# Expert products as filling, norm steps behind the masks, and separate id and gate regions in a delta-rule attention and expert kernel

## The reference, cut to what matters

```python
k_n = k / (norm(k) + 1e-06)
for t in range(S):
    y[:, :, t] = q_t @ state
    state = state + beta_t * outer(k_t, v_t - state @ k_t)
x = (sigmoid(x @ w_gate) * (x @ w_val)) @ w_out        # 3072 x 384, inner 1536
xn = x / (norm(x) + 1e-06);  en = emb / (norm(emb) + 1e-06)
logits = xn @ en.T / tau;    e = argmax(logits)
gate = softmax(logits)[e] (sum + 1e-09)
out = gate * (relu(x @ w1[e]) @ w2[e])                  # inner 1024
```

## Time and profile before

| what | us |
|---|---|
| median of three runs | 1417.88 (1417.28 to 1418.27) |
| the profiled execution, its own time | 1420.6 |
| its span, first to last instruction | 1418.9 |
| start of stages 0, 1, 2, 3 (first product of L976) | 36.27, 68.57, 97.89, 128.30 |
| stages 4 to 23, from one to the next | 39.09 and 39.20 in turn |
| first transposes of the first expert tile (L1215) | 1041.96 |
| first result of DVE from that tile (L749) | 1064.6 |
| one expert tile | 11.6 |

### The profile page before, as it was taken

One profiled execution on the slowest core, in us unless ns is written; L12 is line 12 of the kernel. 1 busy time (PEld: TensorE's weight loads), 2 busy tenths in 40 slices (PEclk: granted clock), 3 DMA queues, 4 the chain that ended last, 5 costly groups with the idle time before them and its releaser, 6 DMA issues.

```text
span 1418.9 us, 28235 instructions
## 1 busy us (share of the span) xinstructions
PE 1324.7 (93%) x11527; PEld 1098.6 (77%) x11527; DVE 581.6 (41%) x1427; ACT 454.6 (32%) x1004; POOL 437.6 (31%) x472
## 2 busy tenths in 40 slices
PE   4899999999999999999999999999559999999996
PEld 4577999999999999999999999999525555555553
DVE  1555444555555555545555555533401111111111
ACT  1445334443434444444434344342101111111110
POOL 4565322333333333323333233312212222222210
PEclk9999999999999999999999999999779999999999
DMA  4232000000000000000000000005231333311100
GB/s 136 72 98 62 18 18 29 13 29 18 30 18 24 13 29 18 19 29 13 29 18 30 15 24 11 24 2 189 87 125 34 119 118 119 121 39 34 33 27 1
DMA packets 42796, 66.89 MB, mean 47 GB/s; under 512 B 6345, under 2 KB 34929, under 8 KB 42672
## 3 DMA queue, kind: packets, MB, share of 16 engines
q1 hardware_dynamic: 36944, 54.19, 11.8%
q0 software_dynamic: 5728, 10.91, 2.6%
HBM read 55.29 MB, written 11.16 MB: 47 GB/s over the span
## 4 chain that ended last, share of the span: by engine, by line
PE 87%; DVE 6%; issue 2%; POOL 2%; ACT 1%; DMA 1%; SPq 0%; POOLq 0%; DVEq 0%
PE ps L1065 23%; PE ps L1228 12%; PE ps L1238 11%; PE ps L1077 8%; PE ps L976 6%; PE ps L1000 3%; PE ps L1030 3%; PE ps L1038 3%; PE ps L1003 2%; DVE MP L550 2%; PE ps L1247 2%; PE ps L1036 2%; PE ps L992 2%; PE ps L960 1%; PE ps L1012 1%
## 5 line engine op out<-in xcount | busy, mean ns | idle before, releaser
L1065 PE MATMUL ps<-xh,wgh 128*128 128x256 f32 x864 | 267.8, 310 | 0.0
L1065 PE MATMUL ps<-xl,wgh 128*128 128x256 f32 x864 | 243.5, 282 | 0.0
L1065 PE MATMUL ps<-xh,wgl 128*128 128x256 f32 x864 | 243.0, 281 | 0.0
L374 POOL TENSOR_TENSOR gl<-sg,gh 128x256 fp32r<-128x256 f32 x144 | 105.8, 735 | 408.2 <-ACT gh L815 408.1
L1228 PE MATMUL ps<-W,xsT 128*128 x372 | 170.2, 608 | 1.9 <-issue 1.0
L1238 PE MATMUL ps<-W,hT 128*128 x496 | 165.1, 486 | 0.9 <-ACT hT L928 0.9
L1065 PEld LDWEIGHTS ps<-xh,wgh 128*128 128x128 f32 x864 | 164.1, 190 | 1.7
L1065 PEld LDWEIGHTS ps<-xl,wgh 128*128 128x128 f32 x864 | 164.7, 191 | 0.5
L1065 PEld LDWEIGHTS ps<-xh,wgl 128*128 128x128 f32 x864 | 163.9, 190 | 0.0
L1238 PEld LDWEIGHTS ps<-W,hT 128*128 128x128 f32 x496 | 94.2, 190 | 73.0 <-issue 15.5
L573 DVE TENSOR_TENSOR sg<-sg,ps 128x256 f32<-128x256 f32 x144 | 60.5, 420 | 216.7 <-ACT sg L811 216.7
(11 more groups left out here) (183 smaller groups left out, 2435.8 us busy)
## 6 DMA issues: line engine op xcount, KB each, us to landing
W<-w_dram SPq DMA_DIRECT2D x16, 1536.0 KB, 11.3
kin<-kv_dram SPq DMA_DIRECT2D x24, 192.0 KB, 2.4
kqT<-qT_dram SPq DMA_DIRECT2D x48, 96.0 KB, 2.5
vin<-kv_dram SPq DMA_DIRECT2D x24, 192.0 KB, 2.3
x_dram<-x2r SPq DMA_DIRECT2D x24, 192.0 KB, 2.0
woT<-woT_dram SPq DMA_DIRECT2D x1, 2304.0 KB, 10.7
stage<-w_gate_dram SPq DMA_DIRECT2D x6, 384.0 KB, 3.1
stage<-w_val_dram SPq DMA_DIRECT2D x6, 384.0 KB, 3.3
```

What stands on the lines that cost most here:

```text
L374: pool.tensor_tensor(gl[n % 2][:, :], gp[n % 2][:, :], gh[n % 2][:, :].bitcast(F32), ALU.subtract).then_inc(gl_ok, 1)
L1065: mm = pe.matmul(ps[n % 2][:, kind * TB:(kind + 1) * TB], w[:, kind, a, cs], v[m % 2][:, a, :], start=(a == 0 and x == 0), stop=(a == KT - ...
```

## The change

Three things are changed.

1. The expert-vector work leaves the opening. Its loads (`emb`, `tau`) count on a semaphore of their own, `emb_in`; POOL's and DVE's first waits no longer include them. DVE's norm of the expert vectors stands in stage 0 between mask 1 and `norm_a`, PE's transposes are put into slot 8 of stage 0, and the 36 products take the place of `warm(3)` in slots 0 to 11 of stage 1, three a slot, with bank 1 in place of bank 7 as their target. POOL's fill of `St` moves from ahead of the norms to behind `scaled_keys`.
2. In each stage with a next group DVE's order changes: `gated(n + 2)` now stands ahead of `norm_b`, and mask 3 ahead of `norm_c`.
3. The triple becomes a pair of ids in `reg_dram` and a gate in a region of its own, `gates_dram`. A pair of groups now has two id scatters and two gate scatters. For the last pair DVE copies the eight logit columns first, chooses, and only then copies the rows; the gate steps move behind the whole table. POOL scatters the ids, waits for row 3 of the table (`row_ok`) and all id scatters, loads ids and gathers the first three tiles; only then it scatters the last gates and loads gates, one load more per tile. SP loads experts 2 and 3 only when the third gather has landed.

```diff
-        sp.dma_start(mI[:, :], mask_d).then_inc(const_in, 16)
...
         load_k(0)
+        sp.dma_start(mI[:, :], mask_d).then_inc(const_in, 16)
...
-        sp.dma_start(emb[:, :], emb_d).then_inc(const_in, 16)
-        sp.dma_start(tau[:, 0:1], tau_d.to_broadcast([P, 1])).then_inc(const_in, 16)
         sp.wait_ge(const_ok, 5)
         load_q(0)
+        sp.dma_start(emb[:, :], emb_d).then_inc(emb_in, 16)
+        sp.dma_start(tau[:, 0:1], tau_d.to_broadcast([P, 1])).then_inc(emb_in, 16)
...
-        sp.wait_ge(pad_ok, 2)
+        sp.wait_ge(pad_ok, 3)
         sp.dma_start(reg_d.rearrange("(p r) c -> p (r c)", p=P), pad[:, :]).then_inc(init_ok, 16)
+        sp.dma_start(gate_d.rearrange("(p r) c -> p (r c)", p=P), pad0[:, :]).then_inc(init_ok, 16)
...
+        sp.wait_ge(wexp[0], 32)
+        sp.sem_inc(w_ready, 1)
+        sp.wait_ge(xs_in[2], 16)
         for e in range(2, SLOTS):
             load_expert(e)
         sp.wait_ge(tab_ok, 1)
-        sp.wait_ge(wexp[0], 32)
-        sp.sem_inc(w_ready, 1)
...
-        def scatter(m):
+        def scatter_ids(m):
             wait(pool, slot_ok, m + 1)
+            for t in range(2 * m, 2 * m + 2):
+                pool.indirect_dma_start(out=reg_d, out_offset=bass.IndirectOffsetOnAxis(ap=slot[:, t:t + 1], axis=0), in_=pay[:, t, :], in_offset=None).then_inc(scat, 16)
+
+        def scatter_gates(m):
             wait(pool, pay_ok, m + 1)
             for t in range(2 * m, 2 * m + 2):
-                pool.indirect_dma_start(out=reg_d, out_offset=bass.IndirectOffsetOnAxis(ap=slot[:, t:t + 1], axis=0), in_=pay[:, t, :], in_offset=None).then_inc(scat, 16)
+                pool.indirect_dma_start(out=gate_d, out_offset=bass.IndirectOffsetOnAxis(ap=slot[:, t:t + 1], axis=0), in_=gate[:, t:t + 1], in_offset=None).then_inc(gscat, 16)
...
-        pool.wait_ge(const_in, CONST_IN)
         pool.wait_ge(const_ok, 6)
         squares(0)
-        pool.memset(St[:, :, :, :], 0.0).then_inc(const_ok, 1)
+        pool.wait_ge(const_in, CONST_IN)
         pool.tensor_copy(mI16[:, :], mI[:, :]).then_inc(const_ok, 1)
         pool.tensor_scalar(mNI[:, :], mI[:, :], -1.0, 0.0, ALU.mult, ALU.add).then_inc(const_ok, 1)
         keys(0)
         scaled_keys(0)
+        pool.memset(St[:, :, :, :], 0.0).then_inc(const_ok, 1)
...
-                scatter(settled(s - 1))
+                scatter_ids(settled(s - 1))
+                scatter_gates(settled(s - 1))
...
-        scatter(settled(NS - 1))
-        scatter(NM - 1)
+        scatter_ids(settled(NS - 1))
+        scatter_gates(settled(NS - 1))
+        scatter_ids(NM - 1)
+        pool.wait_ge(row_ok, 1)
         pool.wait_ge(scat, 16 * NG)
-        pool.wait_ge(x2_out, 32 * NM)
-        pool.wait_ge(tab_ok, 1)
...
+        def load_gates(t):
+            r = pool.value_load(tint[0:1, 3, t:t + 1], min_val=0, max_val=REG - P)
+            pool.dma_start(gts[:, t % 8, :], gate_d[bass.ds(r, P), :]).then_inc(g_in[t % 8], 16)
...
+        pool.wait_ge(x2_out, 32 * NM)
         gather(0)
...
         gather(2)
+        scatter_gates(NM - 1)
+        pool.wait_ge(gscat, 16 * NG)
+        load_gates(0)
+        load_gates(1)
+        load_gates(2)
...
                 gather(k + 3)
+                load_gates(k + 3)
...
-        dve.wait_ge(ssq_ok, 1)
-        root_guess(esc[:, 0:1], esc[:, 1:2])
-        root_step(esc[:, 0:1], esc[:, 1:2], esc[:, 2:3], esc[:, 3:4])
-        root_step(esc[:, 0:1], esc[:, 1:2], esc[:, 2:3], esc[:, 3:4])
-        link(nc.vector.tensor_scalar(esc[:, 2:3], esc[:, 1:2], 1e-6, None, ALU.add))
-        link(nc.vector.reciprocal(esc[:, 4:5], esc[:, 2:3]))
-        nc.vector.tensor_scalar(emb[:, :], emb[:, :], esc[:, 4:5], None, ALU.mult).then_inc(e_ok, 1)
-        link(nc.vector.reciprocal(tau[:, 1:2], tau[:, 0:1]))
         dve.wait_ge(const_ok, CONST_OK)
-        dve.wait_ge(en_ps, 1)
-        nc.vector.tensor_copy(enT[:, :, :], pD[:, 0:KT * E].rearrange("p (a e) -> p a e", e=E)).then_inc(en_ok, 1)
-        dve.wait_ge(woe_ps, 1)
-        nc.vector.tensor_copy(woe[:, :, :], pD[:, 0:NF * E].rearrange("p (f e) -> p f e", e=E)).then_inc(woe_ok, 1)
+
+        def expert_norm():
...
+        def expert_transposed():
+            dve.wait_ge(en_ps, 1)
+            nc.vector.tensor_copy(enT[:, :, :], ps[1][:, 0:KT * E].rearrange("p (a e) -> p a e", e=E)).then_inc(en_ok, 1)
+
+        def expert_weights():
+            dve.wait_ge(woe_ps, 1)
+            nc.vector.tensor_copy(woe[:, :, :], ps[1][:, 0:NF * E].rearrange("p (f e) -> p f e", e=E)).then_inc(woe_ok, 1)
...
+            if s == 0:
+                expert_norm()
             if nxt is not None:
                 norm_a(nxt)
             if g is not None:
                 level_mask(g, 2)
+            if moe:
+                gated(n + 2)
             if nxt is not None:
                 norm_b(nxt)
-            if moe:
-                gated(n + 2)
+            if g is not None:
+                level_mask(g, 3)
             if nxt is not None:
                 norm_c(nxt)
-            if g is not None:
-                level_mask(g, 3)
+            if s == 0:
+                expert_transposed()
...
+            if s == 1:
+                expert_weights()
...
-        rows_out(last)
+        wait(dve, out_ps, NF * NM)
+        wait(dve, x2_out, 32 * last)
+        wait(dve, ssq_ok, 2 * last + 1)
+        for j in range(2):
+            link(nc.vector.tensor_copy(x2r[:, j, HD:], ps[2 + j][:, HD:ROW]))
         choose(last)
-        gate_a(last)
-        gate_b(last)
-        gate_c(last)
+        for j in range(2):
+            nc.vector.tensor_copy(x2r[:, j, 0:HD], ps[2 + j][:, 0:HD]).then_inc(x2_ok, 1)
         rank(last)
         place(last)
-        gate_d(last)
...
-        link(nc.vector.tensor_copy(tint[0:1, 3, :], tid[0:1, 0, :]))
+        nc.vector.tensor_copy(tint[0:1, 3, :], tid[0:1, 0, :]).then_inc(row_ok, 1)
+        dve.wait_ge(row_ok, 1)
...
+        gate_a(last)
+        gate_b(last)
+        gate_c(last)
+        gate_d(last)
...
-                nc.vector.tensor_scalar(ot[r][:, :], ps[5 + r][:, 0:HD], idt[:, (t - 1) % 8, 2:3], None, ALU.mult).then_inc(o_ok, 1)
+                wait(dve, g_in[(t - 1) % 8], 16 * ((t - 1) // 8 + 1))
+                nc.vector.tensor_scalar(ot[r][:, :], ps[5 + r][:, 0:HD], gts[:, (t - 1) % 8, :], None, ALU.mult).then_inc(o_ok, 1)
...
-        act.wait_ge(const_in, CONST_IN)
-        nc.scalar.activation(sq_e[:, :], emb[:, :], ACT.Square, accum_out=esc[:, 0:1]).then_inc(ssq_ok, 1)
...
+        act.wait_ge(emb_in, 32)
+        nc.scalar.activation(sq_e[:, :], emb[:, :], ACT.Square, accum_out=esc[:, 0:1]).then_inc(ssq_ok, 1)
...
+        def expert_transposes():
+            pe.wait_ge(e_ok, 1)
+            for a in range(KT):
+                mm = pe.transpose(ps[1][:, a * E:(a + 1) * E], emb[:, a * P:(a + 1) * P], mI[0:E, 0:E])
+            mm.then_inc(en_ps, 1)
+
+        def expert_weights(f):
+            if f == 0:
+                pe.wait_ge(en_ok, 1)
+                pe.wait_ge(wot_in, 16)
+            for a in range(KT):
+                mm = pe.matmul(ps[1][:, f * E:(f + 1) * E], woT[:, a, f * P:(f + 1) * P], enT[:, a, :], start=(a == 0), stop=(a == KT - 1))
+            if f == NF - 1:
+                mm.then_inc(woe_ps, 1)
...
-        pe.wait_ge(e_ok, 1)
-        pe.wait_ge(kT_ok, 2)
-        for a in range(KT):
-            mm = pe.transpose(pD[:, a * E:(a + 1) * E], emb[:, a * P:(a + 1) * P], mI[0:E, 0:E])
-        mm.then_inc(en_ps, 1)
-        pe.wait_ge(en_ok, 1)
-        pe.wait_ge(wot_in, 16)
-        for f in range(NF):
-            for a in range(KT):
-                mm = pe.matmul(pD[:, f * E:(f + 1) * E], woT[:, a, f * P:(f + 1) * P], enT[:, a, :], start=(a == 0), stop=(a == KT - 1))
-        mm.then_inc(woe_ps, 1)
-        pe.wait_ge(woe_ok, 1)
...
-                    warm(3)
+                    if s == 0 and i == 8:
+                        expert_transposes()
+                    if s == 1 and i < NF:
+                        expert_weights(i)
+                    else:
+                        warm(3)
```

## The result

The changed kernel took 1403.5 us (median of four executions, 1400.6 to 1406.8) against 1418.1 for the kernel before: 0.989 of the time, with a 95% interval of 0.988 to 0.991. The forecast of 1389.5, with a range up to 1400, was too low by 14 us. The profiled execution, the slowest of the four, has a span of 1405.1 us, 13.8 less than that of before. The granted clock over the span is 0.977.

A forecast was written before the change was run, and what follows sets the result against it. TensorE bounds the kernel, with waits in opening, middle stages and handover. Terms -16.6, +0.6, +1.3, +1.1, -3.3 and -11.5 sum to -28.4 us: 1392.2 for the profiled execution, 1389.5 for the median; range 1383 to 1400.

The forecast's parts named there:

- Start, -16.6: Opening: with the expert-vector products gone, the first Gram product starts at about 19.7 us in place of 36.27: -16.6 us.
- Stage 0, +0.6: Stage 0: expert norm delays mask 2, mask 3 follows sooner, mask 4 slightly later: +0.6 us, from -1 to +3.
- Stages 1 and 2, fillings, +1.3: Half-products at 0.107 us replace warm-ups: 0.16 us more per filling, eight fillings not hidden under masks: +1.3 us.
- Rival (a): The clock falls in stage 1, adding 5 to 14 us: 1395 to 1403 us; chance 9%.
- Norm steps in stages 1 and 2, +1.1: Stages 1 and 2: mask 4 now stands behind norm_c's five steps, net +0.6 us in each stage: +1.1 us.
- Stages 3 to 22, -3.3: Middle stages: mask 3 comes 0.3 us earlier in each; nine routed stages give it back: -3.3 us, from 0 to -6.
- rival (c): Middle: norm steps give nothing, mask 4 taking back mask 3's gain: 1393 us; chance 76% together with the likeliest case.
- Doubled scatters, nothing: Middle stages: two more POOL issues in 11 stages, counted at nothing; uncovered they would cost 2.5 us a stage.
- Handover, -11.5: Between last projection and expert tiles: fewer DVE steps and shorter scatter, id load and gather flights: -11.5 us.
- Rival (b): The handover keeps its long flights, since row store and doubled scatters share the queues: 1398 us; chance 7%.
- The Trainium skill's rule on descriptors: Added gate scatters and loads would stretch under DVE's copies; spoke against the change, left out of the sum.
- Behind the last product, 0: End of the program: the expert tiles run at TensorE's pace to the end, untouched by the change: 0 us.

The follow-up runs named there:

- the repetition: The changed kernel itself, unaltered, timed again in rounds on another occasion: 1412.2 us, 0.995 of the kernel before.
- the run with the weights early: The changed kernel with 12-byte id rows, loading weights of experts 2 and 3 without waiting for the third gather: 1404.4 us.

## Why the prediction was wrong, point by point

- **Start, -16.6:** right, in size and reason. It became 18.07, because the casts began at 12.19, 1.3 us earlier than I had them; POOL's squares began 2.7 us earlier, at 5.07, and not the 1.9 that I had.
- **Stage 0, +0.6:** right (+0.32), as far as a stage that differs by 1.1 us from trace to trace can tell. Mask 2 of that stage came 5.35 us behind mask 1 (5 named), and mask 3 2.35 behind mask 2, at the pitch.
- **Stages 1 and 2, fillings, +1.3:** the step that failed, and the largest. I took 0.107 us for a half-product "because stage 1 has a granted clock of 1.00". But that clock was measured with the warm-up products that the change removes. The price of the new work was right while the clock lasted (0.12). Rival (a) named this mechanism, with 5 to 14 us more than the likeliest case; it came at 11 more (42.58 us against the 31.42 of the same stage with the clock up and a warm-up more per group), and at 8.5 in the traces where stage 1 took 39.97. So 9% was far too little for it. The rows at hand would have allowed better: the opening's products, alone on TensorE, had kept the 0.216 pace through all of 15.53 us, which I weighed as "may" only.
- **Norm steps in stages 1 and 2, +1.1:** stage 2 shows +0.32 without a fallen clock; half of the 0.6 I had.
- **Stages 3 to 22, -3.3:** 0.3 a stage in the unrouted ones was right (0.33). The routed ones were to come out even. They lost 0.14, and 0.9 when another step of choose was held. I had named the held step of choose and mask 4 as the next late thing, but put its cost at 0.3 us against 0.3 of gain, with one held step; there are up to three. The term came at -0.69, inside its range of 0 to -6, and outside it in the repetition (rival (c) and beyond).
- **Doubled scatters, nothing:** wrong in one stage of eleven. In stage 24, where no attention work stands between, TensorE waits 1.5 us for the low part behind them. This is read from the trace; no run took them away there.
- **Handover, -11.5:** the DVE steps (3.7 us less, 3.1 counted), the id load (1.96 for 2.2) and the gather (3.16 for 3.1) were right, and so was their reason, by the run with the weights early. The scatter's 3.5 us was the failed step: I took the median of 12-byte rows for rows of 8 bytes. With 12-byte rows it takes 3.54. Rival (b) had the long flights, with the wrong cause.
- **The Trainium skill's rule on descriptors** (SBUF — State Buffer, section "SBUF: two separate sides": a DMA issued by POOL waits while DVE holds the port): left out of the sum, and nothing in the runs asks for it. The added gate scatters took 0.95 to 1.31 us to issue, and with DVE idle the flight was 0.4 us shorter. No run sets a scatter beside a large two-port copy, so the rule itself is not tested.
- **Behind the last product, 0:** -4.55, by a drain that I had not looked at.

Counted by terms, the clock (11 us), the handover (7) and the routed stages (2.6) were too hopeful, and the start (1.5) and the drain (4.55) gave some back: 14.6 us of span.

## What to carry to other kernels

Before work takes the place of warm-up products, ask what the clock does without them: a duration read at 1.00 is only valid while whatever keeps it there stays. A step moved behind one mask stands ahead of the next one; look there for two-input DVE steps that POOL can hold, since such a race gives different times in different executions. When a row that is scattered to DRAM gets narrower, its flight can get longer, so measure it at the new width.

## What the runs showed of the hardware

Scatters of the same 128 rows of 8 bytes landed after 7.6 us with the rows next to one another and after 2.1 with the rows 64 bytes apart. POOL's drain at the end of a program took between 4.3 and 9.6 us; added DMAs moved it, up or down, and what sets it is open. Small steps of DVE with two inputs, 0.17 us long by themselves, took 0.69 and 0.76 us beside an instruction of POOL, one of them in some executions and not in others. With one warm-up product beside each group of products, the same program kept the clock in some executions and lost it in others, 12 us apart.
